# Attention by halves of a chunk: 64 tokens at a time, two heads in the two halves of the partitions

## The reference

```python
for t in range(S):                      # linear attention with decay, per batch and head
    kt, vt, rt = (k[:, :, t], v[:, :, t], r[:, :, t])
    cur = np.einsum('bhd,bhe->bhde', u[None] * kt, vt)
    y[:, :, t] = np.einsum('bhd,bhde->bhe', rt, state + cur)
    state = w[None, :, :, None] * state + np.einsum('bhd,bhe->bhde', kt, vt)
h = x @ w_in                            # 384 -> 2048
g = np.where(h > 0.0, h, np.exp(np.minimum(h, 0.0)) - 1.0)
x2 = g @ w_out                          # 2048 -> 384
# then: the best of 8 experts per token by logits x2 @ w_gate, relu(x2 @ w1) @ w2 of that
# expert, times the softmax value, for at most 384 tokens an expert
```

## Time and profile before

| | |
|---|---|
| median of 3 runs | 410.55 us (410.55 to 410.57) |
| profiled execution | 410.56 us, span 408.8 us |
| TensorE busy | 401.7 us (98%) |
| DVE, ACT, POOL busy | 248.9, 188.6, 234.6 us |
| attention matmuls L1459, L1488, L1517, L1520, L1524, L1528 | 21.6, 6.9, 4.8, 4.3, 7.5, 7.4 us |

### The profile page before, as it was taken

How to read it: one execution, slowest core, us unless ns; L and a number is a source line. 1 busy time by engine, 2 the same in 40 slices (tenths; PEclk the granted TensorE clock), 3 DMA queues, 4 the chain that set the end, 5 groups by cost and what they waited for, 6 DMA issues and landing times.

```text
span 408.8 us, 9457 instructions
## 1 busy us (share of the span) xinstructions
PE 401.7 (98%) x3655; PEld 387.0 (95%) x3655; DVE 248.9 (61%) x585; ACT 188.6 (46%) x411; POOL 234.6 (57%) x239
## 2 busy tenths in 40 slices
PE   8999999999999999999999999999999999999995
PEld 8799799999999999999999999998999999999995
DVE  7787954476567545754573477678747557475532
ACT  4877553233433333334333455463547466465520
POOL 3789865557865785568425334338173753846531
PEclk9999999999999999999999999999999999999999
DMA  7998997113230403011008100646757868568100
GB/s 286 402 396 354 329 366 284 48 73 76 85 120 0 140 21 122 2 69 40 2 1 306 63 0 22 220 186 165 254 179 215 271 191 285 179 199 284 59 33 29
DMA packets 26442, 64.99 MB, mean 159 GB/s; under 512 B 11787, under 2 KB 19509, under 8 KB 24224
## 3 DMA queue, kind: packets, MB, share of 16 engines
q1 hardware_dynamic: 24464, 59.68, 42.4%
q0 software_dynamic: 1792, 4.73, 3.1%
q10 hardware_dynamic: 144, 0.00, 0.0%
HBM read 51.98 MB, written 13.21 MB: 159 GB/s over the span
## 4 chain that ended last, share of the span: by engine, by line
PE 90%; DVE 4%; issue 4%; POOL 1%; ACT 1%; DMA 0%; POOLq 0%; DVEq 0%
PE bank L1438 26%; PE bank L1440 25%; PE bank L1439 25%; PE bank L1459 3%; PE bank L1488 1%; PE bank L1524 1%; PE bank L1528 1%; PE bank L1517 1%; PE bank L1520 1%; PE bank L1615 1%; PE bank L1796 1%; PE bank L1797 1%; PE bank L1800 1%; PE bank L1743 1%; DVE wd_lo L1105 0%
## 5 line engine op out<-in xcount | busy, mean ns | idle before, releaser
L731 POOL TENSOR_TENSOR g_lo<-elu,g_hi 128x256 fp32r<-128x256 f32 x95 | 73.8, 778 | 87.2 <-ACT g_hi L914 86.7
L1438 PE MATMUL bank<-xt,wd_hi 128*128 128x256 f32 x285 | 80.5, 283 | 0.6 <-DVE elu L1235 0.6
L1440 PE MATMUL bank<-xt,wd_lo 128*128 128x256 f32 x285 | 80.4, 282 | 0.0
L1439 PE MATMUL bank<-xt,wd_hi 128*128 128x256 f32 x285 | 80.3, 282 | 0.0
L905 ACT ACTIVATE elu<-elu 128x256 f32<-128x256 f32 x96 | 40.1, 418 | 75.6 <-DVE elu L1227 75.1
L1438 PE MATMUL bank<-wd_hi,g_hi 128*128 128x392 f32 (+1 forms) x192 | 67.4, 351 | 0.0
L1235 DVE SCALAR_TENSOR_TENSOR elu<-elu,bank 128x256 f32<-128x256 f32 x96 | 40.3, 419 | 41.1 <-ACT elu L905 41.1
L1440 PE MATMUL bank<-wd_hi,g_lo 128*128 128x392 f32 (+1 forms) x192 | 65.2, 340 | 0.0
L1439 PE MATMUL bank<-wd_lo,g_hi 128*128 128x392 f32 (+1 forms) x192 | 65.1, 339 | 0.0
L914 ACT CAST g_hi<-elu 128x256 fp32r<-128x256 f32 x96 | 39.0, 406 | 44.1 <-DVE elu L1235 44.1
L1438 PEld LDWEIGHTS bank<-xt,wd_hi 128*128 128x128 f32 x285 | 53.9, 189 | 1.3 <-DVE elu L1235 1.1
(11 more groups left out here) (225 smaller groups left out, 947.6 us busy)
## 6 DMA issues: line engine op xcount, KB each, us to landing
we_raw<-wexp SPq DMA_DIRECT2D x8, 1536.0 KB, 7.5
wd_raw<-wexp SPq DMA_DIRECT2D x8, 1536.0 KB, 6.7
rkt<-rkt SPq DMA_DIRECT2D x12, 512.0 KB, 5.4
nat<-nat SPq DMA_DIRECT2D x9, 672.0 KB, 5.2
wd_raw<-win SPq DMA_DIRECT2D x4, 768.0 KB, 8.1
wd_raw<-wout SPq DMA_DIRECT2D x4, 768.0 KB, 9.1
wo_tr<-wouttr SPq DMA_DIRECT2D x1, 3072.0 KB, 17.3
slots<-blank SPq DMA_DIRECT2D x1, 2702.0 KB, 14.3
```

The costliest lines, as they stand in the source:

```text
L731: nc.gpsimd.tensor_tensor(g_lo[:, f % 4, :], elu[:, f % 2, :], g_hi[:, f % 4, :].bitcast(F32), ALU.subtract).then_inc(s_glo, 1)
L1438: mm(dst, w_hi, x_hi, start=start, stop=False)
L1439: mm(dst, w_hi, x_lo, start=False, stop=False)
L1440: return mm(dst, w_lo, x_hi, start=False, stop=stop)
```

## The change

From chunk 4 on (FIRST) a chunk is two halves of SUB = 64 tokens. Tokens 0 to 63 of a half are put into partitions 0 to 63 for one head of a pair and 64 to 127 for the other (`side` swaps them in every second pair, so that four neighbouring matmuls name the four 64x64 quarters of the array). Scores are made only within a half; the state is carried every 64 tokens, through three state tiles in turn, so there are two outer products, two decays and two state updates a chunk. `nat` comes in a new layout (1408 columns, 1344 before). Banks 4 and 5 become one tensor of two banks, which holds scores and outer products; one mask covers both heads. Small tables in the new layout are made by nine loads. The outer product of chunk c moves from the meeting of c + 1 to the meeting of c, ahead of the scores, and `plan(c)` is written anew; `natural` is at b - 1. The order of features in `xt` and of the rows of `win` follows. `x2_transpose` uses the banks of y.

The core of the diff; `mm` is a matmul, `_halves` functions are new:

```diff
         def plan(c):
             b, before = meeting(c), meeting(c - 1)
-            steps = {"scores": b, "decay": b + (2 if c > 4 else 0), "keys": before + 1, "queries": before + 2,
-                     "mask0": b + (c > 4), "mask1": b + 1 + (c > 4)}
             if c == 2:
-                steps.update(diagonal=2, mask0=4, mask1=6, natural=7, outer=9, back=9, state=10, low=11)
-                del steps["keys"], steps["queries"]
-            elif c < 5:
-                steps.update(rk=before + 3, with_u=before + 4, sum=before + 5, diagonal=before + 5, natural=before + 6)
-                if c == 3:
-                    steps.update(diagonal=8, natural=9, decay=12, outer=13, back=13, low=13, state=14)
+                return dict(scores=b, decay=b, diagonal=2, mask0=4, mask1=6, natural=7, outer=9, back=9, state=10, low=11)
+            if c == 3:
+                return dict(keys=before + 1, queries=before + 2, rk=before + 3, with_u=before + 4, sum=before + 5, scores=b,
+                            diagonal=8, natural=9, mask0=b, mask1=b + 1, decay=12, outer=13, back=13, low=13, state=14)
+            steps = dict(scores=b, outer64=b, state0=b + 1, mask64=b + 2, decay1=b + 2, state1=b + 3,
+                         back=meeting(c + 1), low=meeting(c + 1), sum=b - 1, diagonal=b, natural=b - 1)
+            if c == 4:
+                steps.update(keys=10, queries=11, rk=12, with_u=13, sum=14, diagonal=14, natural=15, decay0=16)
+            elif c == 5:
+                steps.update(rk=b - 5, keys=b - 4, queries=b - 3, with_u=b - 2, decay0=b - 1)
+            elif c == 6:
+                steps.update(keys=b - 6, queries=b - 5, rk=b - 4, with_u=b - 3, sum=b - 2)
+            elif c == 7:
+                steps.update(keys=b - 5, queries=b - 4, rk=b - 3, decay0=b - 2, with_u=b - 2)
             else:
-                steps.update(rk=b - 2, with_u=b - 1, sum=b, diagonal=b, natural=b + 4)
-            if c == 5:
-                steps.update(mask0=b + 1, mask1=b + 4)
-            if c == 6:
-                steps.update(rk=b - 4, with_u=b - 3)
-            if c == 7:
-                steps.update(rk=b - 3)
-            if c > 3:
-                steps.update(outer=meeting(c + 1), state=meeting(c + 1), back=meeting(c + 1), low=meeting(c + 1))
+                steps.update(keys=b - 7, queries=b - 5, decay0=b - 4, rk=b - 3, with_u=b - 2)
             return steps
...
+        def half_state(c, s):
+            return zs[(2 * (c - FIRST) + s) % 3]
+        def side(hp, j):
+            return j ^ (hp & 1)
...
+        def half_block(hp, s):
+            return 4 * (hp & 1) + 2 * s + hp // 2
+        def half_outer(hp, s):
+            at = 2 * C + (2 * s + hp // 2) * 64
+            return score_pair[:, hp & 1, at:at + 64]
+        def half_outers(s):
+            return score_pair[:, :, 2 * C + 2 * s * 64:2 * C + 2 * (s + 1) * 64].rearrange("p b (i e) -> p b i e", i=2)
...
             def load_nat(c):
                 wait_if(sp, s_rku, c - 4)
                 wait_if(sp, s_y, c - 1)
-                sp.wait_ge(s_u, n_states(c - 1))
+                sp.wait_ge(s_u, n_states(c - 1) if c - 2 < FIRST else n_half_states(c - 1, 0))
+                if c >= FIRST:
+                    sp.dma_start(nat[c % 2][:, :], nat2_in[c - FIRST, :, :]).then_inc(s_nat[c % 2], 16)
+                    return
                 lo = RN if c > 2 else KN
...
+                if c == FIRST:
+                    sp.wait_ge(s_y, 3)
+                    sp.wait_ge(s_pwn, 1)
+                    sp.dma_start(u_half, bonus_nat).then_inc(s_half_tab, 16)
+                    for half in range(2):
+                        rows = slice(64 * half, 64 * half + 64)
+                        for b in range(2):
+                            old = pwn[64:128, :].rearrange("p (i m) -> p i m", i=2)
+                            at = 128 * b + 64 * side(b, half)
+                            sp.dma_start(pwn_half[rows, 128 * b:128 * b + 128].rearrange("p (i d) -> p i d", i=2),
+                                         old[:, :, at:at + 64]).then_inc(s_half_tab, 16)
+                        sp.dma_start(ident64[rows, :], ident[rows, rows]).then_inc(s_half_tab, 16)
+                        sp.dma_start(mask64[rows, :], earlier[rows, rows]).then_inc(s_half_tab, 16)
...
             def natural_k1(c):
...
+                if c >= FIRST:
+                    pool.wait_ge(s_half_tab, NHALF)
+                    k = k_nat(c % 2).rearrange("p (b s m) -> p b s m", b=2, s=2)
+                    nc.gpsimd.tensor_tensor(k, k, bc(pwn_half.rearrange("p (b m) -> p b m", b=2).unsqueeze(2),
+                                                     [128, 2, 2, 128]), ALU.mult).then_inc(s_k1n, 1)
+                    return
...
             def diagonal(c):
...
+                if c >= FIRST:
+                    pool.wait_ge(s_half_tab, NHALF)
+                    shape = [128, H, SUB]
+                    nc.gpsimd.tensor_tensor(half_att(c), bc(ident64.unsqueeze(1), shape), bc(bon[p][:, :].unsqueeze(2), shape),
+                                            ALU.mult).then_inc(s_pre[c % 2], 1)
+                    return
...
+                for s in range(2):
+                    c = chunk_for(f"decay{s}", n, f)
+                    if c is not None and half_has_state(c, s) and half_leaves_state(c, s):
+                        decay_half(c, s)
                 for what, piece in (("natural", natural_k1), ("keys", keys), ("queries", queries), ("rk", raw_bonus),
                                     ("with_u", with_u)):
                     c = chunk_for(what, n, f)
-                    if c is not None and (what != "natural" or leaves_state(c)):
+                    if c is not None:
                         piece(c)
...
+            def mask_half(c):
+                shape = [128, 2, 4, SUB]
+                dve.wait_ge(s_pre[c % 2], c // 2 + 1)
+                dve.wait_ge(s_half_tab, NHALF)
+                dve.wait_ge(s_sc, 2 * (c + 1))
+                V.copy_predicated(half_att(c).rearrange("p (b g) t -> p b g t", b=2),
+                                  bc(mask64[:, :].bitcast(U32).unsqueeze(1).unsqueeze(1), shape),
+                                  score_pair[:, :, 0:4 * SUB].rearrange("p b (g t) -> p b g t", t=SUB)).then_inc(s_att, 2)
+            def state_half(c, s):
+                dve.wait_ge(s_u, n_half_states(c, s) + 1)
+                dve.wait_ge(s_sc, 2 * (c + 1))
+                dve.wait_ge(s_y, c)
+                after = by_parity(zs[(2 * (c - FIRST) + s + 1) % 3])
+                if half_has_state(c, s):
+                    dve.wait_ge(s_zw, n_half_decayed(c, s) + 1)
+                    V.tensor_tensor(after, half_outers(s), by_parity(zw[:, :, :]), ALU.add).then_inc(s_z, 1)
+                else:
+                    V.tensor_copy(after, half_outers(s)).then_inc(s_z, 1)
...
+            def outer_halves(c):
+                pe.wait_ge(s_k1n, c + 1)
+                pe.wait_ge(s_z, n_half_states(c, 0))
+                pe.wait_ge(s_att, 2 * c)
+                if c == FIRST:
+                    pe.wait_ge(s_wglo, 1)
+                for s in range(2):
+                    if half_leaves_state(c, s):
+                        for hp in (0, 1, 2, 3):
+                            for j in range(2):
+                                rows = slice(64 * side(hp, j), 64 * side(hp, j) + 64)
+                                key_cols = slice(KN + 64 * half_block(hp, s), KN + 64 * half_block(hp, s) + 64)
+                                v_both = slice(VM + 64 * half_block(hp, s), VM + 64 * half_block(hp, s) + 64)
+                                last = mm(half_outer(hp, s)[64 * j:64 * j + 64, :], nat[c % 2][rows, key_cols],
+                                          nat[c % 2][rows, v_both], start=True, stop=True, skip_group_check=True)
+                        last.then_inc(s_u, 1)
+            def scores_halves(c):
+                p = c % 2
+                pe.wait_ge(s_k1, c + 1)
+                pe.wait_ge(s_r1, c + 1)
+                for s in range(2):
+                    for hp in range(HP):
+                        for j in range(2):
+                            rows = slice(64 * j, 64 * j + 64)
+                            out_rows = slice(64 * side(hp, j), 64 * side(hp, j) + 64)
+                            tokens_of = slice(SUB * s, SUB * (s + 1))
+                            last = mm(half_scores(hp, s)[out_rows, :], k1[p][rows, hp, tokens_of],
+                                      r1[p][rows, hp, tokens_of], start=True, stop=True, skip_group_check=True)
+                last.then_inc(s_sc, 2)
+            def back_halves(c):
+                p = c % 2
+                pe.wait_ge(s_att, 2 * (c + 1))
+                pe.wait_ge(s_xhi, 2 * c)
+                pe.wait_ge(s_xlo, 2 * c)
+                pe.wait_ge(s_z, n_half_states(c, 1))
+                wait_if(pe, s_row, (c - 3) // 2)
+                y = ps_y
+                begun = set()
```

(94 more changed lines are left out.)

62 lines of the change are left out of this document (53 added, 9 removed).

## The result

| | before | changed |
|---|---|---|
| median | 410.55 us (410.48 to 410.57, 4 runs) | 431.44 us (429.77 to 433.59, 4 runs) |
| span of the profiled execution | 408.8 | 429.7 |
| TensorE busy | 401.7 us (98%) | 404.1 us (94%) |

What follows compares the result with a forecast made beforehand. TensorE's instruction stream was taken to bound the kernel. Added waits of 16.7 us, less 0.3 for `att` and 4.5 for cheaper visits, gave +11.9 on 410.56, so 422.5 us, range 416 to 431.

Steps and rivals of the forecast that it cites:

- TensorE is the bound: From 20 us on TensorE's instruction stream alone sets the end; work removed comes off the time, waits add one for one.
- `natural` at b - 1 makes TensorE wait at seven visits: POOL's key scaling ends after TensorE reaches the outer product at q = 22 to 67; together 16.7 us of waits.
- The waits at 29, 43 and 59: At these visits routing steps on DVE make `g_lo` late by over a step; waits of 3.64, 3.12 and 3.12 us.
- My upper bound for the waits: 18.5 us at most, if DVE work put ahead of the late steps added some 0.6 us at each of three visits.
- The clock: Fourth rival: after pauses at 29, 43 and 59 TensorE runs at 1.2 GHz, losing 5 us: 427.5 us; chance 0.10.
- The visits: TensorE's attention work behind fc1 at q = 17 to 75: a full visit gains 0.7 us, together 4.5 us less.
- the second rival: Row halves sharing a PSUM bank don't run beside each other: 1.1 us more a full visit, 430.5 us; chance 0.07.
- The tables, SP's queue, DVE and POOL at nothing: Nine small table loads on SP and the changed masks, state updates, products and decays on DVE and POOL cost nothing.
- What would show it: Seven TensorE waits released by `natural_k1`, 1.1 to 3.7 us each; visits of 2.3 to 2.6 us; clock 9; no `s_half_tab` wait.
- The sign on the clock: TensorE's granted clock must stay at 9.
- the one on the visits: The visit after each wait must take 2.3 to 2.6 us; over 3.3 us the prediction is wrong.
- The rival "TensorE doesn't wait": First rival: POOL's scaled keys are there at the visit, so no wait is added: 405.8 us; chance 0.09.

## Why the prediction was right and wrong

- *TensorE is the bound, and a wait of it is added one for one.* Right: the added wait in the old kernel cost its 10.6 us and more.
- *`natural` at b - 1 makes TensorE wait at seven visits.* Right, place and releaser. The subtraction of two rows of before gave 1.9 for 1.84 and 1.17 for 1.10.
- *The waits at 29, 43 and 59.* The first step that failed: 3.64, 3.12 and 3.12 forecast, 4.4, 4.1 and 4.0 measured in the view, 2.6 us in all. I took the start of `g_lo`(b - 1) from the trace of before and moved only POOL's pieces behind it. But `g_lo`(b - 1) hangs on DVE's routing operations, and the new plan delays these. At 43 and 59 some of them last until a POOL product ends, and the experiment that moved products away brought the starts to 2.9 and 3.1 us. The trace of before already had such a cast, which I had read as DVE's own time; both rows end at 130.7:

```profile
129.79 0.94 DVE L1195 CAST slot_i<-prob 128x2 uint32<-128x2 f32 x1
```

```profile
129.69 1.01 POOL L631 TENSOR_TENSOR rku<-nat 128x384 f32<-128x384 f32 x1
```

At 29 it is another thing. There the small operations are short (the cast 0.17 us), but the plan puts the bonus sum of chunk 6 at b - 2, ahead of them, and it waits for `with_u`:

```profile
93.65 0.56 DVE L1190 TENSOR_REDUCE bon<-rku 128x8 f32<-128x384 f32 x1 [1.03 <-POOL rku L723]
```

Before, that sum came only at 97.39, behind the step. This is read from the trace; no run tests it. My upper bound for the waits (18.5, measured 19.1) named the wrong cause, DVE's state updates.
- *The clock.* The second step that failed, and the larger: the term stood at nothing in the sum, as a rival with a chance of 0.10 and a price of 5 us for the three long pauses, half of each pause. Measured are 7.1 us, behind five waits, two of them of 1.84 us, and the loss is much the same behind a short pause as behind a long one. The earlier trace rows only showed that the clock stays up when TensorE never pauses; that was no reason to give the price so little chance. The Trainium skill (TensorE: Matmul & The Clock Gate, "HAM oscillation — how this bites in real kernels") says that pauses between bursts can put TensorE back to its lower clock, and here the trace agrees: granted clock 0.57 and 0.59 in windows behind such pauses, and 9 in every slice with the pauses filled.
- *The visits.* 4.5 us less forecast, 5.2 measured at full clock (2.45 for 3.25 in a full visit, 2.55 forecast; the 0.12 that I had added for first rounds was too much). 32 records of L1697 and 32 of L1712 take 1.09 us with the changeover, 1.06 forecast. That row halves don't go beside each other in one bank, the second rival from the Trainium skill (TensorEngine Tiling (Array Packing), Restrictions and Gotchas), is not borne out: the quarters that write different partitions of one bank ran side by side, or the visit would have taken 1.1 us more than it did.
- *The tables, SP's queue, DVE and POOL at nothing.* Right for the tables and the loads: no wait of TensorE or POOL for them stands in the views of the visits. Wrong for DVE and POOL, whose busy shares (61% and 57%) I had taken as cover: where their pieces met, `g_lo` came later, the 2.6 us above.
- *What would show it.* The releaser and the seven waits came as listed, though three of them, 4.36, 4.14 and 3.96 us, were over the 3.7. The sign on the clock failed, and with it the one on the visits (2.3 to 2.6 us, none over 3.3): they took 3.99, 3.91 and 3.81 us at 29, 43 and 59.

The sum again with measured terms: 19.6 - 0.65 - 5.2 + 7.1 = 20.9 (the 7.1 is the remainder; the slow work counted piece by piece gives the same). The rival "TensorE doesn't wait" was priced at 405.8; when the experiment took the wait away, it was 405.5. That this is so close is in part luck: the visits gave 0.7 us more than forecast, and the unexplained 0.6 us took about as much.

## What to carry to other kernels

When a matmul moves to an earlier place in the bottleneck's stream, subtract two rows of the trace of before: when its operand's producer gets there, and when the bottleneck does; a step number in a plan is not a time, and an engine at the end of a chain is a step behind. A pause of TensorE can cost more than its length (here 19.6 us of waits brought 7.1 us of work at the lower clock), so price the lower clock as part of the likeliest case and not as a rival. Before a change is given up for its time, see whether its own work got cheaper: here an order written out by hand hid 5 us of gain under 27 of waiting and slow clock.

## What the hardware showed that I had not expected

- Some small DVE operations (2 elements a partition, 0.17 us) last 0.6 to 0.94 us when a POOL product runs, and end with it. Others don't: in the changed kernel L1333 took its 0.17 us at 137.39, inside the product of L714 (137.25 to 138.26). One POOL product of 1 us at the wrong step delayed TensorE by 0.3 to 0.5 us, two engines on, and products at the wrong places in both routing steps by 0.9 to 1.3.
- Pauses of 1.8 to 4.4 us lowered TensorE's clock in most cases and not in all; waits of the same 1.84 us did so at two visits and not at a third of one execution. In the run with the bonus product earlier even a pause of 1.09 us, at q = 22, was followed by a granted clock of 0.67 over 4 us.
